# The channel mix's first product by a seven-product scheme, on 768 tokens at a time

## The chip, the cores and the metric

The kernel runs on one core of one Trainium2 chip. The metric is the device time of one execution in microseconds: 827.92 us is the median of three runs of the kernel before (827.59 to 828.11). The profile is of one further execution on the chip.

## The reference

```python
# attention with pooled queries: q, k, v are (4, 8, 1152, 64)
q_pool = q.reshape(B, H, S // 2, 2, D).mean(axis=3)             # 576 queries a head
scores = scale * np.matmul(q_pool, k.transpose(0, 1, 3, 2))
attn = softmax(scores)                                          # max, exp, sum + 1e-9
x = (attn @ v) as (4, 576, 512)                                 # heads side by side
# channel mix on 2304 tokens of 512
mu, var = mean and variance over the 512
xn = (x - mu) / np.sqrt(var + 1e-06) * g_ln
ch = np.maximum(xn @ w_ch1, 0.0) @ w_ch2                        # 512 -> 2048 -> 512
return x + ch
```

All is float32. Each fp32 product of the score and mix stages is made of three products of high and low parts: an operand a is split into a rounded copy a_hi and the rest a_lo = a - a_hi, and a x b becomes hi x hi + hi x lo + lo x hi.

## The kernel before, in words

Attention runs over 16 pairs of heads. The order of TensorE's and ScalarE's steps in a pair is written out in a string (`PAIR_STEPS`, L75): a letter is a step, the number behind @ the PSUM bank, of which there are eight. S is a block of scores, M a block for the row maxima, L and E the rest of the maxima, SH the turn of the maxima, Z the row sums, PV the values, O the turn of the outputs, KA and KQ the keys' and queries' banks (filled by VectorE's transposes), T the turn of a tile of tokens for the mix. Before a step reuses a bank it waits for whoever read the bank last (`pair_free`, L324). VectorE has a list of its own (`VECTOR_STEPS`, L85): m takes maxima, o scales outputs into `x`, a adds two of the exponential tiles, t makes the low parts of turned tokens. GpSimd adds the exponentials up for the row sums (L447). In pairs 2 to 5 it also splits four slices of the mix's weights (L432, L435), and the rest is split by ScalarE and VectorE in the first chunk.

The mix takes 18 tiles of 128 tokens in six chunks of three (384 tokens). For every one of 16 blocks of 128 hidden columns, TensorE makes `up` (L1051: 12 matmuls of 384 columns, into banks 4 or 5), ScalarE the high part of the Relu (L1101), VectorE its low part (L1122), and TensorE, one block later, `down` (L1064: 9 matmuls of 512 columns, summed over all blocks in banks 0, 1 and 7). All the weights stay in SBUF, split. While a chunk runs, its successor's tokens are normalised (L243), turned by TensorE (L251), scaled by g and rounded by ScalarE (`tokens_hi`, L258), and their low parts made by VectorE (`tokens_lo`, L266). The three turns stand behind blocks 6, 9 and 12 and alternate between banks 6 and 2:

```python
TURN_AT = {6: 0, 9: 1, 12: 2}
```

At a chunk's end VectorE adds the three banks to `x` (L1142), and the sync engine stores the tiles. Every engine works through its instructions in the order in which they are written; between engines there are only semaphores.

## Time and profile before

| | |
|---|---|
| median of the runs | 827.92 us (827.59 to 828.11) |
| profiled execution: span, time | 825.7 us, 827.5 us |
| TensorE busy | 812.1 us (98%), 6620 matmuls |
| VectorE busy | 460.5 us (56%) |
| ScalarE busy | 332.7 us (40%) |
| GpSimd busy | 359.0 us (43%) |
| the mix's first matmul starts | 416.0 us |

The span is the time between the first and the last instruction on the chip, the time of the execution holds a little more on both sides. Busy is the time in which an engine has an instruction under way. For matmuls the mean duration of one is its latency; since they overlap, the pitch (busy time over their number, or the chain's pieces) says what one costs.

### The profile page before, as it was taken

To read this page: it belongs to the slowest core of one execution; us is meant where nothing else is said; L and a number is where in the kernel's file an instruction comes from. 1 tells how busy PE (TensorE), PEld (TensorE's weight loads), DVE (VectorE), ACT (ScalarE), POOL (GpSimd) and SP (SyncE) were. 2 spreads that over 40 slices of the span, in tenths; PEclk is the share of its full clock that TensorE was granted. 3 is DMA by queue.
4 is the path that set the end of the run, shared out by engine and by line. 5 is a ranking of instruction groups with operands and counts; after the bars stand their busy time and mean duration, and the time that the engine had idled before them with its cause. 6 is when DMAs were issued, how large, how long until landed. Compare 5 with 4: busy or idle time off the path is not lost.

```text
span 825.7 us, 16074 instructions
## 1 busy us (share of the span) xinstructions
PE 812.1 (98%) x6620; PEld 686.0 (83%) x6620; DVE 460.5 (56%) x705; ACT 332.7 (40%) x717; POOL 359.0 (43%) x252
## 2 busy tenths in 40 slices
PE   8999999999999999999999999999999999999998
PEld 6777777777777877777789999999999999999997
DVE  7888889889989888977254542232223213122112
ACT  4576556576556667555534321211211121111110
POOL 3988999998889888889720000000000000000000
PEclk9999999999999999999999999999999999999999
DMA  8586534456544456310224310010001001001001
GB/s 196 118 194 143 134 96 93 108 143 143 134 100 97 105 138 142 87 31 2 82 77 128 103 39 0 1 39 1 1 1 39 1 0 39 1 1 39 1 1 39
DMA packets 30840, 58.51 MB, mean 71 GB/s; under 512 B 8240, under 2 KB 18736, under 8 KB 27184
## 3 DMA queue, kind: packets, MB, share of 16 engines
q1 hardware_dynamic: 29296, 57.10, 27.5%
q8 instruction: 53, 0.87, 0.5%
q10 hardware_dynamic: 1472, 0.39, 0.2%
q14 instruction: 19, 0.16, 0.1%
HBM read 52.76 MB, written 4.72 MB: 70 GB/s over the span
## 4 chain that ended last, share of the span: by engine, by line
PE 89%; DVE 7%; ACT 2%; issue 2%; DMA 1%; SPq 0%; POOL 0%; DVEq 0%; ACTq 0%; POOLq 0%
PE banks L1051 24%; PE banks L1064 23%; PE banks L594 16%; PE banks L583 10%; PE banks L527 4%; PE banks L581 3%; DVE pm L878 3%; DVE acc_end L902 2%; PE banks L610 2%; ACT pT L781 1%; PE banks L535 1%; PE banks L621 1%; PE banks L251 1%; PE banks L657 1%; DMA k_in_rows<-in_k_dram 1%
## 5 line engine op out<-in xcount | busy, mean ns | idle before, releaser
L447 POOL TENSOR_TENSOR acc<-acc,pT 128x576 f32<-128x576 f32 x160 | 237.5, 1484 | 23.0
L1051 PE MATMUL banks<-xT,weights 128*128 128x384 f32 x1152 | 216.7, 338 | 0.3 <-DVE weights L1113 0.3
L1064 PE MATMUL banks<-weights,hT 128*128 128x512 f32 x864 | 210.7, 389 | 0.0
L1051 PEld LDWEIGHTS banks<-xT,weights 128*128 128x128 f32 x1152 | 201.5, 188 | 7.0 <-DVE weights L1113 0.8
L1122 DVE SCALAR_TENSOR_TENSOR hT<-banks,hT 128x384 fp32r<-128x384 f32 x96 | 53.5, 558 | 274.4 <-ACT hT L1101 274.4
L781 ACT ACTIVATE pT<-banks 128x576 f32<-128x576 f32 x288 | 171.7, 653 | 37.5 <-PE banks L581 31.5
L1064 PEld LDWEIGHTS banks<-weights,hT 128*128 128x128 f32 x864 | 160.9, 188 | 26.9
L1101 ACT ACTIVATE hT<-banks 128x384 fp32r<-128x384 f32 x96 | 47.2, 492 | 323.5 <-PE banks L1051 323.5
L878 DVE TENSOR_REDUCE pm<-banks 128x2 f32<-128x1024 f32 x128 | 153.2, 1221 | 40.0 <-PE banks L527 39.0
L583 PE MATMUL banks<-qT,kT 64*128 64x288 f32 x1728 | 162.1, 298 | 4.7 <-DVE pm L878 3.5
L583 PEld LDWEIGHTS banks<-qT,kT 64*128 64x128 f32 x1728 | 133.4, 184 | 19.9 <-DVE pm L878 8.8
L594 PE MATMUL banks<-pT,vn 128*64 128x288 f32 x1152 | 145.9, 407 | 0.0
L237 POOL TENSOR_TENSOR rstd<-var_eps,minus_half 128x3 f32<-128x3 f32 x6 | 5.5, 916 | 281.6 <-DVE var_eps L232 281.6
L594 PEld LDWEIGHTS banks<-pT,vn 128*64 128x64 f32 x1152 | 80.3, 137 | 56.3 <-issue 5.6
L581 PE MATMUL banks<-shT,ones 64*128 64x288 f32 x576 | 84.7, 290 | 0.0
L527 PE MATMUL banks<-kT,qT 64*128 64x512 f32 (+1 forms) x384 | 62.6, 365 | 1.5 <-DVE pm L878 1.3
L787 ACT COPY oT<-banks 128x288 f32<-128x288 f32 x32 | 12.8, 399 | 106.9 <-PE banks L594 106.9
L447 POOL TENSOR_TENSOR acc<-pT 128x576 f32<-128x576 f32 x32 | 45.4, 1419 | 23.0 <-ACT pT L781 23.0
L581 PEld LDWEIGHTS banks<-shT,ones 64*128 64x128 f32 x576 | 54.2, 184 | 0.0
L451 POOL TENSOR_TENSOR acc<-acc,acc_end 128x576 f32<-128x576 f32 x32 | 50.7, 1583 | 2.5
L902 DVE TENSOR_TENSOR acc_end<-pT 128x576 f32<-128x576 f32 x32 | 42.0, 1313 | 8.9 <-ACT pT L781 8.6
L527 PEld LDWEIGHTS banks<-kT,qT 64*128 64x128 f32 x384 | 32.5, 184 | 10.5 <-issue 7.1
(89 smaller groups left out, 515.3 us busy)
## 6 DMA issues: line engine op xcount, KB each, us to landing
q_in_rows<-in_q_dram SPq DMA_DIRECT2D x56, 284.0 KB, 6.7
k_in_rows<-in_k_dram SPq DMA_DIRECT2D x56, 284.0 KB, 5.2
vn<-in_v_dram SPq DMA_DIRECT2D x16, 576.0 KB, 5.2
wstage<-in_moe_w_ch_dram SPq DMA_DIRECT2D x32, 256.0 KB, 2.9
out_dram<-x SPq DMA_DIRECT2D x16, 256.0 KB, 2.2
q_in_rows<-in_q_dram SPq DMA_DIRECT2D x4, 256.0 KB, 3.1
k_in_rows<-in_k_dram SPq DMA_DIRECT2D x2, 288.0 KB, 4.1
out_dram<-x SPq DMA_DIRECT2D x4, 128.0 KB, 2.4
```

Source lines behind the costliest of these rows:

```text
L447: nc.gpsimd.tensor_tensor(total, pT[:, h % 2, 0] if kt == 1 else total, pT[:, h % 2, kt], ALU.add).then_inc(chained, 1)
L451: nc.gpsimd.tensor_tensor(total, total, acc_end[:], ALU.add).then_inc(acc_ready, 1)
L527: last = nc.tensor.matmul(dst[:, s, col:col + width], qT[rows, j % 2, 0, t * 128:(t + 1) * 128], kT[rows, j % 2, 0, key:key + width], star ...
L581: last = nc.tensor.matmul(dst, ones[rows], shT[rows, queries], start=False, stop=True)
L583: nc.tensor.matmul(dst, kT[rows, j % 2, a, keys], qT[rows, j % 2, b, queries], start=(a, b) == (0, 0), stop=False)
L594: last = nc.tensor.matmul(dst[s * DH:(s + 1) * DH, 0:HW], vn[:, s, kt], pT[:, h % 2, kt, s], start=kt == 0, stop=kt == KT - 1)
L781: nc.scalar.activation(pT[:, h % 2, kt], pair_banks("S", n)[:, :, 0:HW], ACT.Exp, scale=SCALE).then_inc(exp_done, 1)
L878: nc.vector.tensor_reduce(pm[:, at // GROUPS, :, at % GROUPS], src, AX.X, ALU.max).then_inc(max_taken, 1)
L902: nc.vector.tensor_tensor(acc_end[:], pT[:, h % 2, KT - 2], pT[:, h % 2, KT - 1], ALU.add).then_inc(end_added, 1)
L1051: last = nc.tensor.matmul(ps_h[f % 2][:, 0:CW], weights[:, 2 * f, a, c * 128:(c + 1) * 128], xT[:, par, b, c], start=m == 0, stop=m == len ...
L1064: last = nc.tensor.matmul(ps_y[kk], hT[:, f % 2, a, kk * 128:(kk + 1) * 128], weights[:, 2 * f + 1, b], start=f == 0 and m == 0, stop=f == ...
L1122: nc.vector.scalar_tensor_tensor(out=hT[:, f % 2, 1], in0=ps_h[f % 2][:, 0:CW], scalar=0.0, in1=hT[:, f % 2, 0].bitcast(f32), op0=ALU.max, ...
```

## The change

The mix now takes six tiles at a time (a part, 768 tokens, three parts), as two halves of 384 tokens: `xg_a` and `xg_b`. Two blocks of 128 hidden columns form a unit, eight units a part, 24 in all. With A the transposed weights of a unit, cut into 2 x 2 blocks (128 hidden columns by 256 inputs), and B the tokens, cut into 2 x 2 blocks (256 inputs by 384 tokens), the four blocks of A B come from seven block products (`product`, six matmuls each) of the weight forms A11, S2, A12, S1, S3, S4, A22 with the token forms B11, T2, B21, T1, T3, B22, T4. S and T are sums and differences. GpSimd makes the S's of every unit (`sum_weights`), ScalarE rounds each form (`weights_hi`), VectorE makes the rest (`weights_lo`). The seven products use banks 6 and 7 in turn. VectorE adds them up in SBUF (`mid`, by `middle`): "V", "11", "V5", "V7", "22", "12", "21", of which "11", "12", "21", "22" are the four blocks of hidden values. The Relu's high part comes from ScalarE (`hidden_hi`), the low part from VectorE (`hidden_lo`), and `down` makes its four parts of nine matmuls (k = 0 to 3, banks 0 to 2 for even k, 3 to 5 for odd), one unit later.

The weights don't stay in SBUF: each unit's w_up slice (512 KB) and its two w_down slices (256 KB each) are loaded, and split, again in every part. The token forms of a part (`xf`, 7 forms) are made once, in the unit before and the unit behind the border between parts. The tiles of the first part are turned in attention's pairs 12, 13 and 14, those of the others in units 4, 5 and 6 of the part before, two in each, both into bank 7.

Attention itself: the two turns in a pair move to banks 1 and 0 ahead of SH, Z and PV, GpSimd no longer splits weights, the statistics move to pairs 9 and 10 (three tiles each) and the normalisations to pairs 11 to 13 (two each), and VectorE's last pair has a list of its own.

TensorE at the end of attention's pairs 12 and 13. Before (L594 the values, L560 the turn of the maxima, L610 row sums):

```order
L594 MATMUL banks<-pT,vn 64x288 x17
L560 MATMUL banks<-ident,mx 64x128 [waits max_ready,end_taken]
L560 MATMUL banks<-ident,mx 64x128
L610 MATMUL banks<-acc,tile_ones 64x128 [waits acc_ready,rest_taken]
...
L610 MATMUL banks<-acc,tile_ones 64x96 x2
L594 MATMUL banks<-pT,vn 64x288 [waits v_in,exp_done,rest_taken]
```

Now (L687, L653 and L703 are the same three, L266 is the turn of a tile of tokens):

```order
L687 MATMUL banks<-pT,vn 64x288 x17
L266 MATMUL banks<-ident,xn 128x128 [waits xn_ready,rest_taken]
L266 MATMUL banks<-ident,xn 128x128 x3
...
L653 MATMUL banks<-ident,mx 64x128 [waits max_ready,end_taken]
...
L703 MATMUL banks<-acc,tile_ones 64x128 [waits acc_ready,xg_ready]
...
L703 MATMUL banks<-acc,tile_ones 64x96 x2
L687 MATMUL banks<-pT,vn 64x288 [waits v_in,exp_done,xg_ready]
```

Two turns of four transposes stand in between, and row sums and values wait for `xg_ready`, ScalarE's scaling of the turned tiles.

TensorE in the mix, where it turns tokens. Before (L1051 up, L1064 down, L251 the turn):

```order
L1064 MATMUL banks<-weights,hT 128x512 x8
L251 MATMUL banks<-ident,xn 128x128 [waits xt_ready,xn_ready,x_written]
L251 MATMUL banks<-ident,xn 128x128 x3
L1051 MATMUL banks<-xT,weights 128x384 [waits h_ready,w_ready]
L1051 MATMUL banks<-xT,weights 128x384 x11
```

Now, the end of a unit (L1203 a block product, L1213 down, L266 the turn):

```order
L1203 MATMUL banks<-xf,w1f 128x384 [waits mid_made,w1_lo]
L1203 MATMUL banks<-xf,w1f 128x384 x5
L266 MATMUL banks<-ident,xn 128x128 [waits xn_ready,mid_made]
L266 MATMUL banks<-ident,xn 128x128 x3
L1213 MATMUL banks<-w2f,hT 128x512 [waits h_lo,w2_lo]
L1213 MATMUL banks<-w2f,hT 128x512 x8
L266 MATMUL banks<-ident,xn 128x128 [waits xn_ready,xg_ready]
```

There are two turns in a unit, nine matmuls apart, and the second waits for `xg_ready`. What ScalarE does before it signals that (L1286 `hidden_hi`, L368 `weights_hi`, L1296 the second weights, L282 the scaling):

```order
L1286 ACTIVATE hT<-mid 128x384 [waits down_done,mid_made]
L368 CAST w1f<-w_sums 128x256 [waits product_done,sums_made,w1_in1]
L1286 ACTIVATE hT<-mid 128x384 [waits down_done,mid_made]
L368 CAST w1f<-w_sums 128x256 [waits product_done,sums_made,w1_in1] x2
L368 CAST w1f<-w_stage 128x256 [waits product_done,w1_in1]
L1296 CAST w2f<-w_stage 128x512 [waits down_done,w2_in1]
L282 ACTIVATE xg_b<-banks,g_cols 128x128 [waits x_lo5,x_lo2,tokens_summed,x_lo0,xn_turned]
L282 ACTIVATE xg_b<-banks,g_cols 128x128 x3
```

The second Relu is that of "21", the last sum of a unit; five operations stand between it and the scaling's end.

VectorE behind a border. Before (L266 the low part of turned tokens, L1122 the Relu's low part, L1142 the additions to `x`):

```order
L266 SCALAR_TENSOR_TENSOR xT<-banks,g_cols,xT 128x128 x3
L1122 SCALAR_TENSOR_TENSOR hT<-banks,hT 128x384 [waits h_hi]
L1142 TENSOR_TENSOR x<-banks,x 128x512 [waits down_done] x3
L1122 SCALAR_TENSOR_TENSOR hT<-banks,hT 128x384 [waits h_hi]
L223 BN_STATS stats<-x 128x6
```

Now, the end of the first unit of a part (L1349 `middle`, L373 `weights_lo`, L1354 `hidden_lo`, L1360 the second weights' rest, L240 statistics, L1369 the additions):

```order
L1349 TENSOR_TENSOR mid<-banks,mid 128x384 [waits h_lo,mid_made,product_done]
L373 TENSOR_TENSOR w1f<-w_sums,w1f 128x256 [waits w1_hi]
L1354 SCALAR_TENSOR_TENSOR hT<-mid,hT 128x384 [waits h_hi]
L373 TENSOR_TENSOR w1f<-w_sums,w1f 128x256 [waits w1_hi]
L373 TENSOR_TENSOR w1f<-w_stage,w1f 128x256 [waits w1_hi]
L1360 TENSOR_TENSOR w2f<-w_stage,w2f 128x512 [waits w2_hi]
L240 BN_STATS stats<-x 128x6 [waits x_written]
L240 BN_STATS stats<-x 128x6 x2
L1369 TENSOR_TENSOR x<-banks,x 128x512 [waits down_done]
L1369 TENSOR_TENSOR x<-banks,x 128x512 x2
L1354 SCALAR_TENSOR_TENSOR hT<-mid,hT 128x384 [waits h_hi]
L1369 TENSOR_TENSOR x<-banks,x 128x512 [waits down_done]
```

The additions came right behind the chunk's last Relu; now they stand behind eight more operations, and TensorE's `down` of that unit waits for them (`summed`).

The diff, cut to its core:

```diff
-    CT = 3
-    CHUNKS = ALL_TILES // CT
-    CW = CT * 128
+    CT = 6
+    PARTS = ALL_TILES // CT
+    CW = CT // 2 * 128
+    FP = FC // 2
+    UNITS = PARTS * FP
+    FORMS = 7
+    HC = DC // 2
+    W_RING = 9
...
-                  "S@6 M@4 S@0 O@6 E@3 L@0 PV@2 KQ@4 KA@6 T@4 T@5 SH@3 Z@1 PV@0")
+                  "S@6 M@4 S@0 O@6 E@3 L@0 PV@2 T@1 T@0 KQ@4 KA@6 SH@3 Z@1 PV@0")
...
-    TURNS = {PAIRS - 2: (0, 1), PAIRS - 1: (2,)}
+    TURNS = {PAIRS - 4: (0, 1), PAIRS - 3: (2, 3), PAIRS - 2: (4, 5)}
...
+        def sum_weights(eng, vector, u):
+            vector.wait_ge(w1_in[u % 2], 16 * (u // 2 + 1))
+            wait(vector, w1_lo, FORMS * (u - 2) + S4 + 1)
...
+            eng.tensor_tensor(s1, a21, a22, ALU.add).then_inc(sums_made, 1)
+            eng.tensor_tensor(weight_block(u, S3), a11, a21, ALU.subtract).then_inc(sums_made, 1)
+            vector.wait_ge(sums_made, 4 * u + 1)
+            eng.tensor_tensor(s2, s1, a11, ALU.subtract).then_inc(sums_made, 1)
+            vector.wait_ge(sums_made, 4 * u + 3)
+            eng.tensor_tensor(weight_block(u, S4), a12, s2, ALU.subtract).then_inc(sums_made, 1)
...
+        def last_pair_vector(dve):
+            j = PAIRS - 1
+            for i in (T1, T2):
+                sum_tokens(nc.vector, dve, 0, i)
+            tokens_hi(dve, nc.vector.tensor_copy, 0, T2)
+            tokens_hi(dve, nc.vector.tensor_copy, 0, T1)
+            tokens_lo(nc.vector, dve, 0, T2)
+            tokens_lo(nc.vector, dve, 0, T1)
+            add_end(dve, 2 * j)
+            sum_tokens(nc.vector, dve, 0, T3)
+            sum_tokens(nc.vector, dve, 0, T4)
+            take_end(j + 1)
+            scale_outputs(j - 2)
+            add_end(dve, 2 * j + 1)
+            for i in range(FORMS):
+                weights_lo(0, i)
+                if i == S2:
+                    take_end(j + 2)
+                    scale_outputs(j - 1)
+            for i in (B22, T3, T4):
+                tokens_lo(nc.vector, dve, 0, i)
...
+            def product(u, i):
...
+                elif i == 0:
+                    pe.wait_ge(mid_made, mid_made_by(u - 1, "21"))
...
+                elif i == 2:
+                    pe.wait_ge(first_copied, u + 1)
+                elif i > 2:
+                    pe.wait_ge(mid_made, mid_made_by(u, ("V", "11", "V5", "22")[i - 3]))
+                terms = [(a, b, c) for c in range(HC) for a, b in ((0, 0), (0, 1), (1, 0))]
...
+            for u in range(UNITS):
+                turns = turned_in(u)
+                product(u, 0)
+                if u:
+                    down(u - 1, 0)
+                product(u, 1)
+                product(u, 2)
+                if u:
+                    down(u - 1, 1)
+                product(u, 3)
+                if u == 0:
+                    tensor_step(pe, "Z", PAIRS - 1)
+                product(u, 4)
+                if u:
+                    down(u - 1, 2)
+                product(u, 5)
+                product(u, 6)
+                if turns:
+                    pe.wait_ge(mid_made, mid_made_by(u, "12"))
+                    turn_tokens(*turns[0], banks[:, 7])
+                if u:
+                    down(u - 1, 3)
...
+                if turns:
+                    pe.wait_ge(xg_ready, CT * turns[0][0] + turns[0][1] + 1)
+                    turn_tokens(*turns[1], banks[:, 7])
...
+            for u in range(UNITS):
+                n, p = at_border(u), u % FP
+                following = u // FP + 1
+                middle(u, "V")
+                next_lo(u, 0)
...
+                middle(u, "12")
+                next_lo(u, 3)
+                hidden_lo(u, 1)
+                middle(u, "21")
+                next_lo(u, 4)
+                hidden_lo(u, 2)
+                next_lo(u, 5)
+                next_lo(u, 6)
+                if u == 0:
+                    take_end(PAIRS + 2)
+                    scale_outputs(PAIRS - 1)
+                second_lo(2 * u + 1)
+                if following < PARTS:
+                    if p < 2:
+                        dve.wait_ge(x_written, PAIRS)
+                        for kk in range(CT // 2):
+                            statistics(following, CT // 2 * p + kk)
```

## Rows read from the trace of the kernel before

**Rows 1.** The page: busy time of TensorE, and its granted clock in 40 slices.

```profile
PE 812.1 (98%) x6620; PEld 686.0 (83%) x6620; DVE 460.5 (56%) x705; ACT 332.7 (40%) x717; POOL 359.0 (43%) x252
...
PEclk9999999999999999999999999999999999999999
```

**Rows 2.** Groups: line, engine, operation, shapes, count | busy us, mean ns | idle before.

```profile
L1051 PE MATMUL banks<-xT,weights 128*128 128x384 f32 x1152 | 216.7, 338 | 0.3 <-DVE weights L1113 0.3
L1064 PE MATMUL banks<-weights,hT 128*128 128x512 f32 x864 | 210.7, 389 | 0.0
```

**Rows 3.** Window of the second chunk: stretch, length, busy us by engine, clock, DMA.

```profile
483.40:550.70 67.30, 67.30 (x350) 61.51 (x349) 17.55 (x42) 10.96 (x28) 0.85 (x1) 1.00 0.03 12
```

**Rows 4.** Chain of waits, in the mix: start us, us, what.

```profile
450.42 2.08 PE banks L1051 x12
454.55 2.08 PE banks L1051 x12
...
482.30 4.08 PE banks L1064 x18
...
549.68 4.08 PE banks L1064 x18
```

**Rows 5.** Timeline at the handover: start us, us, engine, line, what.

```profile
407.79 7.93 POOL L447 TENSOR_TENSOR acc<-acc,pT 128x576 f32<-128x576 f32 x5
...
411.04 1.14 ACT L258 ACTIVATE xT<-banks,g_cols 128x128 fp32r<-128x128 f32 x4 [0.24 <-PE banks L251]
...
415.79 1.42 POOL L451 TENSOR_TENSOR acc<-acc,acc_end 128x576 f32<-128x576 f32 x1
416.04 2.35 PE L1051 MATMUL banks<-xT,weights 128*128 128x384 f32 x12
```

**Rows 6.** Timeline at the end of the mix.

```profile
817.68 4.24 PE L1064 MATMUL banks<-weights,hT 128*128 128x512 f32 x18
817.88 0.49 ACT L1101 ACTIVATE hT<-banks 128x384 fp32r<-128x384 f32 x1 [3.63 <-PE banks L1051]
```

**Rows 7.** Groups of VectorE, by shape.

```profile
L1122 DVE SCALAR_TENSOR_TENSOR hT<-banks,hT 128x384 fp32r<-128x384 f32 x96 | 53.5, 558 | 274.4 <-ACT hT L1101 274.4
...
L1113 DVE TENSOR_TENSOR weights<-wstage,weights 128x512 fp32r<-128x512 f32 x28 | 18.0, 685 | 2.9 <-ACT weights L1093 2.9
...
L223 DVE BATCH_NORM_STATS2 stats<-x 128x6 f32<-128x512 f32 x18 | 12.1, 683 | 0.0
```

**Rows 8.** Timeline of VectorE: two weight rests without a wait between.

```profile
428.93 1.27 DVE L1113 TENSOR_TENSOR weights<-wstage,weights 128x512 fp32r<-128x512 f32 x2
```

**Rows 9.** Groups of ScalarE, by shape.

```profile
L1101 ACT ACTIVATE hT<-banks 128x384 fp32r<-128x384 f32 x96 | 47.2, 492 | 323.5 <-PE banks L1051 323.5
...
L1093 ACT CAST weights<-wstage 128x512 fp32r<-128x512 f32 x28 | 16.1, 625 | 0.0
...
L733 ACT CAST kT<-banks 128x128 fp32r<-128x128 f32 x16 | 4.6, 285 | 0.0
```

**Rows 10.** A group of GpSimd.

```profile
L457 POOL TENSOR_TENSOR kT<-pT,kT 128x1152 fp32r<-128x1152 f32 x2 | 5.3, 2628 | 4.1 <-ACT pT L756 4.1
```

**Rows 11.** Line L902, VectorE beside GpSimd: ns min/median/max, first and last start.

```profile
L902 DVE TENSOR_TENSOR acc_end<-pT x32: 757/1376/1881, 31.2 to 406.4; 128x576 f32<-128x576 f32 x32
```

**Rows 12.** Chain of waits at the end of pair 13.

```profile
361.45 0.22 PE banks L560 x4
361.67 1.05 PE banks L610 x24
362.72 4.37 PE banks L594 x36
```

**Rows 13.** Chain of waits: the first values of pairs 1, 2 and 3.

```profile
61.39 4.52 PE banks L594 x36
...
85.89 4.52 PE banks L594 x36
...
110.67 4.52 PE banks L594 x36
```

More of the change, by code:

```diff
@@ L256, in tokens_hi @@
             nc.scalar.wait_ge(xn_turned, CT * n + kk + 1)
-            for c in range(DC):
-                last = nc.scalar.mul(xT[:, par, 0, c, kk * 128:(kk + 1) * 128], bank[:, c * 128:(c + 1) * 128],
-                                     g_cols[:, c:c + 1])
-            last.then_inc(xt_hi, 1)
-        def tokens_lo(n, par, kk, bank):
-            nc.vector.wait_ge(xt_hi, CT * n + kk + 1)
-            for c in range(DC):
-                at = slice(kk * 128, (kk + 1) * 128)
-                last = nc.vector.scalar_tensor_tensor(
-                    out=xT[:, par, 1, c, at], in0=bank[:, c * 128:(c + 1) * 128], scalar=g_cols[:, c:c + 1],
-                    in1=xT[:, par, 0, c, at].bitcast(f32), op0=ALU.mult, op1=ALU.subtract)
-            last.then_inc(xt_ready, 1)
+            for i in (B11, B21, B22):
+                wait(nc.scalar, x_lo[i], n)
@@ new lines, in scale_tokens @@
+            wait(nc.scalar, tokens_summed, 4 * n)
+            if n == 0 and kk >= CT // 2:
+                nc.scalar.wait_ge(kq_turned, PAIRS)
+                nc.scalar.wait_ge(ka_turned, PAIRS)
+            half, at = (xg_a, xg_b)[kk // 3], slice(kk % 3 * 128, (kk % 3 + 1) * 128)
+            for c in range(DC):
+                last = nc.scalar.mul(half[:, c, at], bank[:, c * 128:(c + 1) * 128], g_cols[:, c:c + 1])
+            last.then_inc(xg_ready, 1)
+        B11, T2, B21, T1, T3, B22, T4 = range(FORMS)
@@ new lines, in pooled_attention_channel_mix, with sum_tokens @@
+        A11, S2, A12, S1, S3, S4, A22 = range(FORMS)
+        BLOCK_SUMS = (S1, S3, S2, S4)
+        def sum_tokens(eng, vector, n, i):
+            low, high = slice(0, HC), slice(HC, DC)
+            count = 4 * n + (T1, T2, T3, T4).index(i)
+            vector.wait_ge(xg_ready, CT * (n + 1))
+            if i == T1:
+                wait(vector, x_lo[T3], n)
+                out, a, b = token_sums[:, 0], xg_b[:, low], xg_a[:, low]
+            elif i == T2:
+                wait(vector, x_lo[T4], n)
+                out, a, b = token_sums[:, 1], xg_b[:, high], token_sums[:, 0]
+            elif i == T3:
+                vector.wait_ge(x_lo[T1], n + 1)
+                out, a, b = token_sums[:, 0], xg_b[:, high], xg_b[:, low]
+            else:
+                vector.wait_ge(x_lo[T2], n + 1)
+                out, a, b = token_sums[:, 1], xg_a[:, high], token_sums[:, 1]
+            wait(vector, tokens_summed, count)
+            eng.tensor_tensor(out, a, b, ALU.subtract).then_inc(tokens_summed, 1)
@@ L972, in attention_vector @@
+                if j == PAIRS - 6:
                     moments_of(0)
                     variance_eps(0)
[L974 to L976 removed]
+                if PAIRS - 5 <= j < PAIRS - 2:
+                    for kk in range(2):
+                        normalize(0, 2 * (j - PAIRS + 5) + kk)
                 if j == PAIRS - 2:
[L978 to L982 removed]
@@ L1009, in mix_sync @@
[L1009 to L1020 removed]
+                    dve.wait_ge(scored, KT * 2 * (PAIRS - 1))
@@ new lines, in pooled_attention_channel_mix, with mid_made_by, turned_in, at_border @@
+        PRODUCT_BANK = (6, 7, 6, 7, 6, 7, 6)
+        MADE = ("V", "11", "V5", "V7", "22", "12", "21")
+        BLOCKS = ("11", "12", "21", "22")
+        BLOCK_AT = (2, 3, 4, 1)
+        def mid_made_by(u, what):
+            return len(MADE) * u + MADE.index(what) + 1
+        def turned_in(u):
+            n, p = divmod(u, FP)
+            return [(n + 1, kk) for kk in range(2 * p - 8, 2 * p - 6)] if 4 <= p < 7 and n + 1 < PARTS else []
+        def at_border(u):
+            n, p = divmod(u, FP)
+            return n + 1 if p == FP - 1 and n + 1 < PARTS else None
@@ L1021, in mix_sync, with behind_border, load_second_weights, send @@
+        def behind_border(u):
+            return u // FP if u % FP == 0 and u else None
+        def mix_sync(sp):
+            def load_second_weights(m):
+                wait(sp, w2_lo, m - 1)
+                sp.dma_start(w2_stage[:, m % 2], w2_v[:, m % FC]).then_inc(w2_in[m % 2], 16)
+            def send(tile):
                 c, t = tile // TILES, tile % TILES
@@ new lines, in send @@
+                return 16
+            sp.wait_ge(pv_done, HALVES)
+            for m in range(2):
+                load_second_weights(m)
+            sent = 0
+            for u in range(UNITS):
+                if u + 2 < UNITS:
+                    load_first_weights(sp, u + 2)
+                if u + 1 < UNITS:
+                    for m in (2 * u + 2, 2 * u + 3):
+                        load_second_weights(m)
+                if behind_border(u):
+                    sent += sum(send(CT * (u // FP - 1) + kk) for kk in range(CT))
@@ L1171, in _ @@
                 attention_vector(dve)
+                last_pair_vector(dve)
                 mix_vector(dve)
```

530 lines of the change are left out of this document (321 added, 209 removed).

## The prediction

> **What bounds the kernel now.** I began with the shares and slices of the page: TensorE is busy 98% of the span and its granted clock is 9 tenths or more in every slice [rows 1]. The costliest groups say on what: the channel mix's first product (L1051, 1152 matmuls of 384 columns) and its second (L1064, 864 of 512) hold 216.7 and 210.7 us [rows 2]. The window of one chunk says who else works there: in 67.3 us TensorE is busy for 67.3, VectorE for 17.6, ScalarE for 11.0 [rows 3]. So in the mix TensorE alone sets the time, and the others have room. The chain of waits gives pitches: twelve first-product matmuls take 2.08 us (0.174 each), eighteen second-product ones 4.08 (0.227 each), and a chunk 67.38 [rows 4], of which 16 x (2.085 + 2.04) = 66.0 is products and the rest three turns of four transposes, 0.46 each. The whole mix is 416.04 to 821.92, 405.9 us [rows 5, 6].
>
> **What is removed.** Seven block products of 6 matmuls for eight: 42 matmuls a unit of 256 hidden columns and 384+384 tokens, 24 units, 1008 for 1152. 144 x 0.174 = 25.0 us less on TensorE. The second product keeps its 864. TensorE's own work in the mix becomes 1008 x 0.1737 + 864 x 0.227 + 12 turns x 0.46 + 2.2 (last row sums and turns of outputs) = 378.9 us. Were it never to wait, the change would gain 27 us. So the question is only what it waits for.
>
> **Prices of what is added.** VectorE: 384 wide 0.56 us, 512 wide 0.69 [rows 7]; 256 wide lies between, 0.42. Without a wait between them two of 512 take 1.27, so each costs 0.09 less in a row [rows 8]: 0.47, 0.60, 0.34. ScalarE: 0.49 for 384, 0.62 for 512, 0.28 for 128 [rows 9], so 0.39 for 256, again some 0.09 less in a row; a turned tile scaled in four pieces takes 1.14 [rows 5]. GpSimd: 1.59 for 576 [rows 5], 2.63 for 1152 [rows 10], so about 0.75 for 256 and 1.85 for 768. Most new operands lie in SBUF; L1113 and L1093 read SBUF too, so the prices hold for them.
>
> **One steady unit.** TensorE's order is P0 D0 P1 P2 D1 P3 P4 D2 P5 P6 D3 (P 1.04 us, D 2.04): P5 ends at 12.38, P6 at 13.42, the unit at 15.46. Products have two banks, so every product waits for the sum that empties its bank. In the first half there is room (V at 4.3, "11" at 5.4, V5 at 8.5, "22" by 11.1, wanted at 12.4). The tight chain is the last: P5's end is seen 0.2 later (a product's end to its Relu, [rows 6]), "12" 0.56, ScalarE's Relu and the weight copy behind it 0.8, VectorE's weight rest and hidden rest 0.81, "21" 0.56: done at 15.4, and P0 of the next unit wants bank 6 at 15.46. I charge 0.15 us for each of 13 plain units, 2 us. Bounds: 0, and 0.5 a unit.
>
> **The units that turn tokens** (p = 4 to 6 of the first two parts, six in all). Both turns go to bank 7, and the second waits until ScalarE has scaled the first. ScalarE works in order: behind "21" (15.4) come a Relu (0.40), three weight copies (0.93), the second weights' copy (0.52) and only then the scaling (1.14): 18.4. TensorE, with one turn and D3 behind P6, is there at 15.9 and waits 2.6 us. Six times: 15.6 us. With the copies at their 128-wide price it is 2.2 each, with everything at the full price of one 3.2: 13 to 19. Before, successive turns had different banks and three first products between them. This term alone takes over half of the gain.
>
> **The two borders between parts.** In the last unit of a part VectorE makes four low parts of 768 (0.9 each) between its sums; "22" is then ready only at 12.5 and "21" at 16.1: 0.8 us a border. In the unit behind it VectorE's queue is "21", three weight rests, a hidden rest, the second weights' rest: 18.35; then three statistics (1.8, [rows 7]) and only then the additions that empty banks 0 to 2. The first is done at 20.9. D0 of the next unit, for these banks, wants it at 16.5: 4.4 us at the first border; 2.6 at the second, which has no statistics to take. Together 8.6 (5 to 12).
>
> **The handover from attention.** In the last pair VectorE had almost nothing; now it makes sums, high and low parts of 768-wide operands beside GpSimd, which adds until 417.2 [rows 5]. Beside GpSimd such an instruction of 576 took between 0.76 and 1.88 us, median 1.38 [rows 11]. By the median it reaches the seven weight rests at 412 and, with the last three token forms, V of unit 0 only near 421.7 (before's clock), while P2 ends at 419.5: 2.9 us. In unit 0 no D lies between the products, so they run at VectorE's pace: 1.3 us more. D0 waits for the last scaled outputs, which stand behind the weight rests: 2.8 us. Sum 7.0. Bounds: 3 (no contention) and 11.
>
> **Attention.** Three times two token turns now take banks 1 and 0, ahead of row sums (bank 1) and values (bank 0), which then wait for ScalarE's scaling. Now the row sums start 0.22 behind the maxima's turn and the values 1.05 later [rows 12]. With the turns, ScalarE's oT copy and two scalings (0.36 + 1.14 + 1.07 from 361.5, the end of the values) end at 364.1, so the values start at 364.3 instead of 362.7: 1.7 us for pairs 12 and 13; in pair 14, which already had two turns on other banks, 0.85; the turn in pair 15 is gone, -0.45. GpSimd's early weight splits go: their pairs took 24.78 us and the one before them 24.50 [rows 13], 4 x 0.28 = 1.1 gained. Moved statistics and normalisations: +0.3. Net +3.0 (0.5 to 5).
>
> **Sum.** 378.9 + 2 + 15.6 + 8.6 + 7.0 = 412.1 against 405.9: +6.2. With attention's 3.0, +9.2. The end (three additions, stores) is the same. On the profiled execution, span 825.7 and time 827.5, that gives 836.7; the median of the runs is 827.9, so 837.1. 0.2% is 1.7 us, about what a measurement of this kernel can tell from no change.
>
> **A rule beside it.** [Rows 11] show one VectorE form between 0.76 and 1.88 us while GpSimd works. The Trainium skill, SBUF — State Buffer, section on SBUF's two separate sides, says that a VectorE instruction with two SBUF inputs and a GpSimd one exclude each other for a whole instruction. The spread agrees. By that rule a steady unit, too, can lose one GpSimd instruction: a rival below.
>
> **Rivals.**
> - *The lock falls into the tight chain.* GpSimd makes four weight sums a unit, 3.0 us. They wait for a 512 KB load that is asked for some 3 us into the unit; I place them at 8 to 11, where VectorE has a microsecond to spare. If they start at 12 to 14, the two rests in the tight chain wait for one sum: 0.75 in each of 23 units, +14 net of the slack: 851. For it: [rows 11]. Against: the place. 12%.
> - *The clock falls.* It is at its upper level throughout [rows 1], and TensorE hardly waited in the mix [rows 3], so nothing here shows what a wait of 4 us does. If one border and the handover each brought a unit at 1.2 GHz, a unit's work costs 15.5 more: up to 31, at half of that 852. The Trainium skill, TensorE: Matmul & The Clock Gate, part on the HAM clock gate, says that an idle spell throttles TensorE to half; the two long waits are where that would bite. 8%.
> - *Faster.* Instructions between SBUF and SBUF are shorter than I price them. At half the price "21" is ready at 14.3, the turn costs 0.6 instead of 2.6 (-12), the borders 3.5 less, the handover 4 less: 817.6. It becomes faster than before from about half of that effect, instructions a quarter shorter. Against: L1113 and L1093 read SBUF and follow the PSUM line. 6%.
> - *Half of it covered.* The handover and attention's 10 us hide behind GpSimd's or ScalarE's present idle time: 827, no change. For it: VectorE idles most of the last pair. Against: order of the queues. 6%.
> - Forecast, 829.6 to 846: 68%.
>
> Slower is the forecast, the lock and the clock, and the edge of the half-covered case: 89%. Faster 7% (its rival and 1% of the half-covered), same 4%. The range 829 to 852 takes in the lock and leaves out the faster case, the half-covered one and half of the clock's, 16% in all.
>
> **What would show it.** TensorE's matmuls in the mix 1008 and 864; its turns in the mix waiting on ScalarE's scaling six times, 2 to 3 us each; second-product matmuls waiting on VectorE's output additions by 4.4 and 2.6 us behind units 8 and 16; plain units of 15.5 to 15.7 us; a first product that waits on `mid` at the start; attention's values later by 1.7 in two pairs. If the plain units take over 16 us, the tight chain is longer than I read; if the turn waits are under 1 us, my ScalarE prices are wrong, and with them the sign.

## The result: 866.3 us for 828.0, slower by 4.6%

The changed kernel took 866.3 us (863.9 to 867.9), the kernel before 828.0 (827.6 to 828.5): ratio 1.046, interval 1.043 to 1.049. I had forecast 837.1 in a range of 829 to 852. The direction was right, the size was not: of the 38 us I had 9.

The page of after (span 863.8 us, its own time 865.5), the lines that answer to [rows 1, 2]:

```profile
PE 811.1 (94%) x6476; PEld 672.0 (78%) x6476; DVE 660.2 (76%) x1011; ACT 418.9 (49%) x948; POOL 454.8 (53%) x347
...
PE   8999999999999999999689988887998888899998
...
PEclk9999999999999999999889999999999999999999
...
L1213 PE MATMUL banks<-w2f,hT 128*128 128x512 f32 x864 | 220.7, 402 | 8.9 <-DVE x L1369 6.3
L1203 PE MATMUL banks<-xf,w1f 128*128 128x384 f32 x1008 | 201.2, 347 | 15.8 <-DVE mid L1349 15.6
```

The products are as few as the change says, 1008. But TensorE is busy 94% where it was 98, its row has 8s and a 6 in the mix's half, and the 864 second-product matmuls, which the change does not touch, hold 220.7 us instead of 210.7 [rows 2]. So there are two losses: waits, and the same work done more slowly. The waits of TensorE (line and tile, the engine and line waited for, total, times, longest):

```profile
PE banks L1203 <- DVE mid L1349: 15.6, 8, 7.1
PE banks L266 <- ACT xg_a L282: 9.4, 4, 2.4
PE banks L1213 <- DVE x L1369: 6.3, 2, 3.9
PE banks L266 <- ACT xg_b L282: 4.7, 2, 2.4
PE banks L1213 <- DVE x L799: 2.6, 1, 2.6
```

That is 38.6 us of waits: the six turns (9.4 + 4.7), the additions (6.3), the last outputs (2.6), the sums of blocks (15.6). All but three of them, short waits for the sum "22" near the borders, stand where I had looked for one. The other loss shows in the table by stretch (length, busy time of each engine, granted clock, DMA):

```profile
426.00:436.00 10.00, 5.58 (x38) 5.06 (x39) 7.90 (x13) 1.92 (x5) 5.26 (x6) 0.66 0.19 58
436.00:444.00 8.00, 4.22 (x24) 3.37 (x22) 5.85 (x14) 3.87 (x10) 0.00 (x0) 1.00 0.09 28
444.00:449.00 5.00, 4.86 (x16) 4.08 (x17) 2.94 (x5) 0.00 (x0) 0.02 (x1) 0.66 0.52 157
...
510.00:529.80 19.80, 16.98 (x89) 15.12 (x90) 11.30 (x24) 8.45 (x25) 3.07 (x4) 1.00 0.18 54
529.80:534.80 5.00, 5.00 (x20) 4.46 (x19) 1.19 (x3) 2.01 (x7) 1.11 (x2) 0.66 0.52 157
534.80:548.00 13.20, 13.03 (x68) 11.53 (x66) 6.84 (x15) 3.33 (x9) 1.76 (x3) 1.00 0.09 21
548.00:554.00 6.00, 3.81 (x13) 3.58 (x14) 2.72 (x6) 4.55 (x14) 1.55 (x1) 0.72 0.40 132
```

The clock is at its upper level (2.4 GHz) except in spells of half clock (1.2 GHz) that begin in or right behind a wait: the wait of 7.1 us at the handover, the 2.6 at 444.1, and the second and the third turn wait (529.5, 550.2), not the first (510.5). Such spells stand at nine places of the mix, some 3.4 us long each and twice that at the handover. In the first behind a turn, P0 and D0 took from 529.99 to 534.72, 4.73 us for work of 3.1.

The mix lasts from 419.88 to 860.62, 440.7 us instead of my 412.1; it starts 3.84 later than before (forecast 3.0).

**Three places in the trace.** A unit that turns tokens, first VectorE, then ScalarE, then TensorE (start, us, instruction, idle before):

```profile
504.58 0.56 DVE L1349 TENSOR_TENSOR mid<-banks,mid 128x384 f32<-128x384 f32 x1 [0.54 <-PE banks L1203]
506.02 0.42 DVE L373 TENSOR_TENSOR w1f<-w_sums,w1f 128x256 fp32r<-128x256 f32 x1 [0.89 <-ACT w1f L368]
506.36 0.55 DVE L1354 SCALAR_TENSOR_TENSOR hT<-mid,hT 128x384 fp32r<-128x384 f32 x1
506.83 0.55 DVE L1349 TENSOR_TENSOR mid<-banks,mid 128x384 f32<-128x384 f32 x1
```
```profile
507.42 0.53 ACT L1286 ACTIVATE hT<-mid 128x384 fp32r<-128x384 f32 x1 [1.43 <-DVE mid L1349]
...
508.75 0.61 ACT L1296 CAST w2f<-w_stage 128x512 fp32r<-128x512 f32 x1
509.27 1.13 ACT L282 ACTIVATE xg_a<-banks,g_cols 128x128 f32<-128x128 f32 x4
```
```profile
510.46 0.66 PE L266 MATMUL banks<-ident,xn 128*128 128x128 f32 x4 [2.36 <-ACT xg_a L282]
```

VectorE idles 0.89 us for ScalarE's weight copy while "21" is next but two; everything behind "21" on ScalarE is late by it and by the two rests. The handover, VectorE beside GpSimd, and TensorE:

```profile
419.63 1.54 DVE L373 TENSOR_TENSOR w1f<-w_stage,w1f 128x256 fp32r<-128x256 f32 x1
421.09 4.07 DVE L373 TENSOR_TENSOR w1f<-w_sums,w1f 128x256 fp32r<-128x256 f32 x3
...
427.34 2.34 DVE L337 TENSOR_TENSOR xf<-token_sums,xf 128x768 fp32r<-128x768 f32 x2
429.71 0.56 DVE L1349 TENSOR_TENSOR mid<-banks,mid 128x384 f32<-128x384 f32 x1
```
```profile
414.46 8.00 POOL L542 TENSOR_TENSOR acc<-acc,pT 128x576 f32<-128x576 f32 x5
422.54 1.48 POOL L546 TENSOR_TENSOR acc<-acc,acc_end 128x576 f32<-128x576 f32 x1
...
426.68 1.32 POOL L360 TENSOR_TENSOR w_sums<-w_stage,w_sums 128x256 f32<-128x256 f32 x1
```
```profile
430.42 2.26 PE L1203 MATMUL banks<-xf,w1f 128*128 128x384 f32 x6 [7.10 <-DVE mid L1349]
...
444.14 3.83 PE L1213 MATMUL banks<-w2f,hT 128*128 128x512 f32 x9 [2.60 <-DVE x L799]
```

A weight rest costs 0.42 where GpSimd is idle (row 506.02), here 1.36 to 1.54. V, the first sum, comes at 429.7, not at the 425.5 that my 421.7 makes with the start 3.84 later. GpSimd's row sums, which ended at 417.2 before (421.0 with the same shift), last until 424.0, and weight sums follow until 428.0. And the border behind unit 7:

```profile
566.91 1.85 POOL L313 TENSOR_TENSOR token_sums<-xg_b 128x768 f32<-128x768 f32 x1 [6.91 <-issue]
568.93 1.81 POOL L313 TENSOR_TENSOR token_sums<-xg_a,token_sums 128x768 f32<-128x768 f32 x1 [0.17 <-POOL token_sums L313]
```
```profile
568.97 2.18 DVE L1354 SCALAR_TENSOR_TENSOR hT<-mid,hT 128x384 fp32r<-128x384 f32 x1
571.07 0.55 DVE L1349 TENSOR_TENSOR mid<-banks,mid 128x384 f32<-128x384 f32 x1
```
```profile
571.77 1.29 PE L1203 MATMUL banks<-xf,w1f 128*128 128x384 f32 x6 [2.33 <-DVE mid L1349]
...
593.81 0.47 PE L1213 MATMUL banks<-w2f,hT 128*128 128x512 f32 x1 [3.94 <-DVE x L1369]
```

A hidden rest, 0.55 elsewhere, takes 2.18 beside GpSimd's token sum, in the tight chain right ahead of "21". I had priced that border's chain with GpSimd idle.

### The profile page after: what moved, and what is told of

Read it like the earlier page. It is cut to its first block and busy times, and to the rows that moved or that the text cites. A ratio compares the mean times of both kernels' runs of the same rounds, so it can differ in the third digit from the quotient of the medians.

```text
span 863.8 us, 17118 instructions
## 1 busy us (share of the span) xinstructions
PE 811.1 (94%) x6476; PEld 672.0 (78%) x6476; DVE 660.2 (76%) x1011; ACT 418.9 (49%) x948; POOL 454.8 (53%) x347
## 5 line engine op out<-in xcount | busy, mean ns | idle before, releaser
L1213 PE MATMUL banks<-w2f,hT 128*128 128x512 f32 x864 | 220.7, 402 | 8.9 <-DVE x L1369 6.3
L1203 PE MATMUL banks<-xf,w1f 128*128 128x384 f32 x1008 | 201.2, 347 | 15.8 <-DVE mid L1349 15.6
L1203 PEld LDWEIGHTS banks<-xf,w1f 128*128 128x128 f32 x1008 | 181.9, 193 | 28.6 <-issue 22.8
L1213 PEld LDWEIGHTS banks<-w2f,hT 128*128 128x128 f32 x864 | 166.4, 195 | 39.6 <-issue 7.1
L1286 ACT ACTIVATE hT<-mid 128x384 fp32r<-128x384 f32 x96 | 50.5, 526 | 270.0 <-DVE mid L1349 270.0
L1349 DVE TENSOR_TENSOR mid<-banks,mid 128x384 f32<-128x384 f32 x168 | 93.2, 555 | 77.3 <-PE banks L1203 73.8
L676 PEld LDWEIGHTS banks<-qT,kT 64*128 64x128 f32 x1728 | 133.5, 185 | 18.8 <-DVE pm L987 7.6
L687 PE MATMUL banks<-pT,vn 128*64 128x288 f32 x1152 | 145.9, 407 | 0.0
L355 POOL TENSOR_TENSOR w_sums<-w_stage 128x256 f32<-128x256 f32 x23 | 18.5, 804 | 207.8 <-DMA w_stage<-in_moe_w_ch_dram 207.8
L687 PEld LDWEIGHTS banks<-pT,vn 128*64 128x64 f32 x1152 | 80.3, 137 | 56.2 <-issue 5.6
L373 DVE TENSOR_TENSOR w1f<-w_sums,w1f 128x256 fp32r<-128x256 f32 x96 | 46.5, 486 | 61.3 <-ACT w1f L368 61.3
L1354 DVE SCALAR_TENSOR_TENSOR hT<-mid,hT 128x384 fp32r<-128x384 f32 x96 | 64.6, 673 | 2.9 <-ACT hT L1286 2.6
```

What stands on the lines that cost most here:

```text
L676: nc.tensor.matmul(dst, kT[rows, j % 2, a, keys], qT[rows, j % 2, b, queries], start=(a, b) == (0, 0), stop=False)
L687: last = nc.tensor.matmul(dst[s * DH:(s + 1) * DH, 0:HW], vn[:, s, kt], pT[:, h % 2, kt, s], start=kt == 0, stop=kt == KT - 1)
L1203: last = nc.tensor.matmul(banks[:, PRODUCT_BANK[i], 0:CW], w1f[:, m % W_RING, a, c], xf[:, i, b, c], start=at == 0, stop=at == len(terms) - 1)
L1213: last = nc.tensor.matmul(banks[:, k % 2 * (CT // 2) + kk], hT[:, k, a, tokens], w2f[:, (2 * u + k // 2) % 4, b], start=p == 0 and k < 2 a ...
L1349: nc.vector.tensor_tensor(mid[:, at], banks[:, PRODUCT_BANK[i], 0:CW], mid[:, other], ALU.add).then_inc(mid_made, 1)
L1354: nc.vector.scalar_tensor_tensor(out=hT[:, k, 1], in0=mid[:, BLOCK_AT[k]], scalar=0.0, in1=hT[:, k, 0].bitcast(f32), op0=ALU.max, op1=ALU. ...
```

## Experiments

All are edits of the changed kernel; times are medians, with the range in brackets; n = 4 for each.

**1. Each suspected wait by itself.** Scaling the first turned tile ahead of the weight copies:

```diff
                 next_hi(u, 3)
+                if turns:
+                    scale_tokens(*turns[0], banks[:, 7])
                 hidden_hi(u, 2)
 ...
                 second_hi(2 * u + 1)
-                if turns:
-                    scale_tokens(*turns[0], banks[:, 7])
```


> ScalarE scales the first turned tile of a unit ahead of the Relu of '21' instead of four copies behind it; all else as in the changed kernel. Theory (the wait is one of order): the six waits of 2.36 us before the second turn vanish, 14.2 us, and with them the stretches at the lower clock that follow two of the three in each part, some 1.5 us each of four: 866.3 becomes 846 to 850. Rival (ScalarE and VectorE have too much to do in these units, the order is not at fault): the wait turns up again before P0 or P2 of the next unit, and the time falls by less than 5 us.

846.2 us (845.7 to 846.8): 20.1 faster. The turn waits, 14.1 us, are gone, and the 1872 matmuls hold 414.1 us instead of 421.9, since fewer of them run at half clock (mean clock 0.99 for 0.98). Of that, 3.8 us came back as waits for block sums (19.4 for 15.6).

The additions to `x` ahead of "12", and the statistics a unit later:

```diff
+                if behind_border(u):
+                    dve.wait_ge(down_done, 4 * u - 1)
+                    for kk in range(CT // 2):
+                        add_outputs(CT * (u // FP - 1) + kk)
                 if n:
                     tokens_lo(nc.vector, dve, n, T1)
                 middle(u, "12")
```


> VectorE adds output tiles 0 to 2 right behind '22' in the unit behind a border, and takes the statistics one unit later (units 1 and 2 of a part instead of 0 and 1). Theory: the waits of 3.94 and 2.36 us before D0 of units 9 and 17 shrink to under 0.5, '21' of that unit comes 0.8 later (the additions lie before '12'), the lower clock behind both goes (1.5 us each): 6 to 9 us less than 866.3. Rival: the additions only move the wait to P0, less than 3 us.

862.3 us (860.9 to 863.9): 4.0 faster. The waits of 3.94 and 2.36 us went, but 1.15 us came at the sum that now stands behind the additions, and 0.3 to 0.6 where the statistics went: all waits together fell by 1.1 us only. The larger part of the gain lies in the matmuls, 418.5 us for 421.9.

GpSimd's token sums for the next part held back until "21":

```diff
                 if n:
+                    pool.wait_ge(mid_made, mid_made_by(u, "21"))
                     sum_tokens(nc.gpsimd, pool, n, T3)
```


> At the two borders GpSimd waits for '21' before it makes the token sums T3 and T4. Theory (GpSimd's instruction blocks the hidden rest L1354, which took 2.18 us there instead of 0.55): the hidden rest in the tight chain is back at 0.55, the wait before P0 of units 8 and 16 falls from 2.33 and 2.37 us to about 0.8, so 3 us less, and 1.5 more at the second border where the lower clock followed: 861 to 864. Rival (VectorE's own four low parts of 768 make the wait): no change at these places.

867.2 us (865.2 to 867.4): no gain. TensorE and VectorE of this run:

```profile
571.36 1.29 PE L1204 MATMUL banks<-xf,w1f 128*128 128x384 f32 x6 [0.23 <-DVE mid L1350]
...
581.45 2.35 PE L1204 MATMUL banks<-xf,w1f 128*128 128x384 f32 x12 [2.58 <-DVE mid L1350]
```
```profile
575.50 2.07 DVE L373 TENSOR_TENSOR w1f<-w_sums,w1f 128x256 fp32r<-128x256 f32 x1
577.49 2.05 DVE L373 TENSOR_TENSOR w1f<-w_stage,w1f 128x256 fp32r<-128x256 f32 x1
```

The wait of 2.33 fell to 0.23, so GpSimd's sum was its cause. But GpSimd's work now lies beside the next unit's rests (2.07 for 0.42) and the wait came back there as 2.58. The expectation took the wait for gone where it only moved.

Issuing V's operands first, the last three token rests behind it:

```diff
-            for i in (B22, T3, T4):
-                tokens_lo(nc.vector, dve, 0, i)
 ...
                 middle(u, "11")
+                if u == 0:
+                    tokens_lo(nc.vector, dve, 0, T3)
```


> In unit 0 VectorE makes the low parts of T3, B22 and T4 between the sums instead of ahead of V. Theory (order of VectorE's queue): V comes at 426 instead of 429.7, the wait before P3 falls from 7.1 to about 3.4; the low parts then lie between the sums, 2 us of it come back before P4 to P6: 1 to 3 us less than 866.3, 1.5 of which from the clock. Rival (the handover is bound by the amount of work, not its order): no change within 1 us.

861.4 us (861.0 to 864.8): 4.9 faster, more than either theory; the 7.10 fell to 3.42.

**2. The clock by itself.** Dummy transposes of the identity into a free bank fill the waits (20 at each turn, 60 at the handover, 18 to 32 at the borders); no operation of the kernel changes.

```diff
+                    pe.wait_ge(mid_made, mid_made_by(u, "21"))
+                    filler(20, 6)
                     pe.wait_ge(xg_ready, CT * turns[0][0] + turns[0][1] + 1)
```


> TensorE fills its long waits with transposes whose result nobody reads: 20 before each second turn, 60 before P3 of unit 0, 18 before P0 of units 8 and 16, 32 and 18 before D0 of units 8 and 16. No wait is made shorter. Theory (part of the loss is the clock, which was at its lower level for some 3.4 us behind eight of the waits): the granted clock stays at 1.00, and every product runs at 0.174: 10 to 13 us less than 866.3, the waits themselves as long as before. Rival (the granted clock falls for another reason than idle time, or the work behind a wait was slow for lack of data): the time stays within 3 us or rises by the fillers that overrun the waits.

855.5 us (855.0 to 856.3), mean clock 0.997: 10.8 faster with every wait still there: the six turning units take 19.05 to 19.07 us each, where after has 19.05 to 19.12 for four of them and 20.64 and 20.86 for the two in which a spell lies. This is what the half-clock spells cost, net: one spell is left (at 443.4), and at the borders some of the dummy work runs longer than the wait that it fills.

**3. The contention by itself.** GpSimd's additions for the last pair run over 8 of 288 columns, so its row sums are left out but for these.

> GpSimd's additions for the row sums of the last pair run over 8 of 288 columns (the row sums of that pair are left out but for those), all else as in the changed kernel. Theory (GpSimd's instructions block VectorE's in the last pair and push V of unit 0 from 422 to 429.7): VectorE's instructions there fall to their times alone, 0.95 us for 768 and 0.42 for 256, the wait before P3 of unit 0 falls from 7.1 us to under 1, the lower clock there goes: 8 to 11 us less than 866.3. Rival (ScalarE's copies or the loads are late, or VectorE simply has too much to do): the wait stays above 4 us.

857.2 us (856.6 to 859.2): 9.1 faster. VectorE's line that answers to the row at 421.09:

```profile
418.19 1.09 DVE L373 TENSOR_TENSOR w1f<-w_sums,w1f 128x256 fp32r<-128x256 f32 x3
```

Three rests take 1.09 us instead of 4.07, V starts at 422.4 instead of 429.7, and the wait of 7.10 is gone.

**4. What a product is worth.** P0 issued twice, so eight products:

> The first product of every unit is issued twice (the same result is written again), so that TensorE has eight products a unit again: 144 matmuls more. Theory (outside its waits the mix is TensorE's, and a product not made is worth its full time): 24 x 1.05 = 25 us more, less some 1 us each in the two waits for the output additions: 888 to 892. Rival (the units run at VectorE's or ScalarE's pace, the seven-product scheme saves little): 5 to 12 us more.

877.9 us (876.5 to 881.3): 11.6 slower, not 25. Plain units grew by the full 1.07 us (15.71 to 16.78), but a longer TensorE stretch swallows waits (the additions' 6.3 us fell to 4.3, the block sums' 15.6 to 13.4, the outputs' 2.6 to 1.5) and the mean clock rose from 0.98 to 0.992.

**5. Together.** Edits e1, e2 and e6:

> The early scaling, the early additions with later statistics, and V first in unit 0, together. Theory: the three act on different waits, so they add: 20.1 + 4.0 + 2 less than 866.3, about 840. Rival (they share VectorE's and ScalarE's time): under 20 less.

838.8 us (838.6 to 840.3), 27.5 less than the changed kernel, where the three gave 20.1, 4.0 and 4.9 alone. Then unit 0's weight rests 4 to 6 behind V, and the last outputs scaled right behind "21":

> This is the kernel with the three reorderings (838.8 us) with one more, in unit 0 alone: the first-product weight rests 4 to 6 are taken after V instead of ahead of it, and the last pair's outputs are scaled right behind middle 21 instead of behind weight rests 4 to 6 of the next unit. Theory (what is left of the handover's loss is VectorE's queue, since TensorE waited 3.41 us before P3(0), then 1.69, 0.96 and 2.58 us): V comes three rests of about 1.5 us each earlier only if GpSimd does not stretch what is left, so P3's wait falls to 1 to 2 and the 2.58 to about 1.2; 834 to 837. Rival (GpSimd's sum, not VectorE's order, sets the time of the last of these waits): at most 1 us less, 837.5 to 839.

834.9 us (834.7 to 835.5), 3.9 less. The borders rearranged instead (turns in units 3 to 5, GpSimd's six token rests given to VectorE, its first two token sums earlier and the other two behind "21"):

> The kernel with the three reorderings (838.8 us) with the borders (units 7 to 9 and 15 to 17) rearranged: the tokens are turned in units 3 to 5 of a part instead of 4 to 6, the statistics all stand in unit 1, GpSimd takes the sums T1 and T2 in unit 6 ahead of its weight sums and T3, T4 behind middle 21 of unit 6, and VectorE instead of GpSimd takes the rests of B22, T3 and T4, spread over units 7 and 8. Theory (the borders' waits, 6.6 us at each, are the next part's preparation crowded into the tail of one unit, on two engines that stretch each other): they fall to 1 to 2 us at each border, 829 to 832. Rival (the work only moves, as it did when GpSimd's sums alone were put later): within 2 us of 838.8.

837.6 us (836.0 to 839.3), 1.2 less, where I expected 7 to 10: the rival. Waits moved from the sum "21" to V5 and "22" (1.72 and 1.36 us), which now stood behind token rests on VectorE. All waits for block sums fell by 3.4 us (20.9 to 17.5), but the clock did not gain (mean 0.992 for 0.994). Both:

> Both of these on top of the three reorderings. If the losses of handover and borders are separate queues, the two gains add: 826 to 829, so level with the kernel before (828.0), which would put the scheme's whole deficit of 38 us on order. Rival (a rest of the deficit is work, not order: 2.5 us of pitch in plain units, 3.8 in attention, the handover's own sums): 830 to 835.

835.3 us (833.7 to 835.8), not 826 to 829. In all of these I had moved rests about, and each time a sum stood behind one. So the next kernel put the sums first (diff against e11, units past 0):

```diff
                     hidden_lo(u, 0)
+                    middle(u, "V5")
                     if n:
                         tokens_lo(nc.vector, dve, n, T2)
-                middle(u, "V5")
 ...
                 middle(u, "22")
+                if n:
+                    tokens_lo(nc.vector, dve, n, B21)
                 middle(u, "12")
+                middle(u, "21")
+                if behind_border(u): ...  # the additions to x
                 next_lo(u, 3)
                 hidden_lo(u, 1)
-                middle(u, "21")
```


> The kernel with handover and borders reordered (835.3 us), with VectorE's sums of blocks put ahead of its rests. In every unit 21 stands right behind 12, ahead of the first-product weight rest 3 and the hidden rest 1 (VectorE waited there 0.89 us on ScalarE with the next sum behind it). In the crowded units V5, V7 and 22 stand ahead of B21's rest, the second weight's rest and the additions to x, and in unit 0 V5, V7 and 22 ahead of all that belongs to unit 1. No operation is added or removed. Theory (all of what is left is sums queued behind rests that nobody needs yet): TensorE's waits of 3.40, 1.75 and 0.85 us in unit 0 go to 1.5 together, the borders' 5.3 us each to 1 to 2, and the half clock behind them goes: 820 to 825, faster than the kernel before (828). Rival (a rest of the deficit is engine time, not order: the rests moved behind the sums are then late themselves, as in the two late-sums and border kernels): 832 to 837.

**818.2 us** (817.9 to 819.2), ratio to the kernel before 0.988 (0.987 to 0.990): 1.2% faster than the kernel before, with an interval clear of 1, and faster than the changed kernel, and below my forecast for it. Its page and its waits:

```profile
PE 795.2 (97%) x6476; PEld 662.6 (81%) x6476; DVE 662.3 (81%) x1017; ACT 418.8 (51%) x948; POOL 445.8 (55%) x341
...
PEclk9999999999999999999999999999999999999999
...
L1220 PE MATMUL banks<-w2f,hT 128*128 128x512 f32 x864 | 213.1, 392 | 0.1
L1210 PE MATMUL banks<-xf,w1f 128*128 128x384 f32 x1008 | 195.1, 339 | 8.0 <-DVE mid L1356 6.7
```
```profile
PE banks L1210 <- DVE mid L1356: 6.7, 10, 1.4
PE banks L1210 <- DVE w1f L385: 1.1, 1, 1.1
```

Waits of 38.6 us became 7.8, and the same 1872 matmuls take 408.2 us instead of 421.9. The work is that of the changed kernel, but six token rests are now VectorE's instead of GpSimd's (x1017 and x341 for x1011 and x347), as in the two border orders above.

**6. The last questions.** P0 twice again, in this order:

> The kernel with the sums ahead (818.2 us) with the first of the seven block products issued twice (the second start overwrites the first, nothing else changes), so eight products of columns in the new order. It measures what a product is worth on TensorE where little waits: in the changed kernel the same edit cost 11.6 us, since waits took up the rest. Theory (order was the whole loss): 24 units by 1.07 us, less the 6.7 us of waits that a longer TensorE stretch can swallow: 19 to 25 us, so 837 to 843. Rival (another engine is by now close to being the bound, VectorE at 76% of the span): 8 to 15 us, 826 to 833.

836.9 us (836.5 to 837.2): 18.7 slower, at the edge of the first theory (837) and clearly not the rival's 826 to 833. The starts of P0 in two plain units, of e12 and of e13:

```profile
758.41 1.21 PE L1210 MATMUL banks<-xf,w1f 128*128 128x384 f32 x6
...
774.00 1.21 PE L1210 MATMUL banks<-xf,w1f 128*128 128x384 f32 x6
```
```profile
756.71 1.21 PE L1211 MATMUL banks<-xf,w1f 128*128 128x384 f32 x6
...
773.35 1.21 PE L1211 MATMUL banks<-xf,w1f 128*128 128x384 f32 x6
```

15.59 and 16.64: 1.05 us a unit, 25.2 in all, less what the waits took up (7.8 us in e12, 2.5 here). The rest, 1.2, I did not trace.

And in the changed kernel one line alone, "21" right behind "12":

```diff
                 middle(u, "12")
+                middle(u, "21")
                 next_lo(u, 3)
                 hidden_lo(u, 1)
-                middle(u, "21")
```


> The changed kernel (866.3 us) with one line moved in the units: the sum 21 right behind 12, ahead of the first-product weight rest 3 and the hidden rest 1. Nothing else of the reorderings. In the changed kernel 12 starts at 504.58 us and 21 at 506.83, with VectorE waiting on ScalarE between; product 6 is done about 505.7. Theory (the chain 12, 21, Relu, copies, scaled tokens sets the turn waits): each turn wait of 2.36 us loses about 1.1 us, 6.7 us over the six units, and with waits of 1.3 us the clock holds there, 3 to 6 us more: 853 to 860. Rival (product 6 ends too late, so 21 can't start earlier): 864 to 867.

842.6 us (842.4 to 845.7): **23.7 faster**, well past both ranges. VectorE, TensorE and the stretch of the second turn in this run:

```profile
503.50 0.56 DVE L1349 TENSOR_TENSOR mid<-banks,mid 128x384 f32<-128x384 f32 x1 [0.50 <-PE banks L1203]
```
```profile
507.14 0.66 PE L266 MATMUL banks<-ident,xn 128*128 128x128 f32 x4 [1.18 <-ACT xg_a L282]
```
```profile
523.00:541.00 18.00, 16.83 (x88) 14.99 (x87) 10.68 (x23) 7.85 (x24) 3.06 (x4) 1.00 0.19 59
```

The first row is "21": it starts 13.73 us into its unit (P0 at 489.77) where after has 15.01 (506.83, P0 at 491.82). The turn waits halved (14.1 to 7.0 us in all). By units, the two profiled executions differ by 19.8 us: 10.8 in the six turning units, 6.0 at the borders (the wait of 2.33 for "21" is gone there, and 1.6 of it is back in the unit behind), 1.8 at the handover and 1.2 in the ten plain units (15.71 to 15.59). Of these, 10.0 are in the same matmuls: 214.9 and 197.0 us, where after has 220.7 and 201.2. With turn waits of 1.2 us in the same places the clock stayed up. I had allowed 3 to 6 us for it, and nothing for borders and plain units. The other 4 us lie between executions: the profiled one was e14's slowest (845.7 us, mean clock 0.990), the other three took 842.4 to 842.7 at 0.996.

## Why the prediction was wrong

The mix took 28.6 us more than forecast. By the prediction's own terms, each from the pitches of the units in the traces of after and of e4, in which dummy work keeps the clock up; the first row is not measured but taken over, and the others are what is left above it:

| term | forecast | measured | with the clock held (e4) |
|---|---|---|---|
| products, turns, last rows | 378.9 | 378.9 | 378.9 |
| plain units | 2.0 (0.15 each) | 2.5 (0.25 each) | 2.5 |
| six turning units | 15.6 | 19.5, of it waits 14.1 | 16.1 |
| borders (units 7 to 9, 15 to 17) | 8.6 | 24.3, of it waits 13.5 | 18.8 |
| handover | 7.0 | 15.6, of it waits 11.0 | 14.3 |
| attention | +3.0 | +3.8 | |

Three steps failed. The sum held the clock at its upper level throughout; it took the sum "21" at the borders to be made beside an idle GpSimd (waits of 2.33 and 2.37 us for 0.8); and it put the first wait at the handover at 2.9 us where it was 7.10. In the trace of after TensorE works 30.7 us at half clock, which loses 15.3; waits are 7.4 longer than forecast (4.9 at the borders, 4.0 at the handover, 1.5 less at the turns); the pitch of 15.71 for 15.46 makes 3.7. That is 26.4 of the 28.6; 2.2 are unplaced. The net cost of the clock is less than 15.3: with it held, some waits that the slow work had hidden are back, so e4 gained 10.8.

- **Work removed:** right. 1008 products, 1.05 us for a block product in a plain unit (e12 against e13).
- **Engine prices and the plain unit:** right. 0.42, 0.55 and 0.69 on VectorE, 0.40, 0.61 and 1.13 on ScalarE, for the 0.42, 0.56, 0.69, 0.39, 0.62 and 1.14 that [rows 7 to 9] gave. Only the Relu was longer, 0.53 for 0.49.
- **Turn waits:** right in mechanism and size, 2.36 us each for 2.6 (my own terms add up to 2.5). e1 took them away.
- **The clock.** The sum held every second at the upper level and gave the clock a rival at 8%, tied to the two longest waits. It falls behind waits of 2.4 us too, though not behind each, and it ran through turning units, borders and handover: 10.8 us by e4, 10.0 in the matmuls of e14. That [rows 1] have no low slice says nothing on this, since TensorE hardly waited there.
- **The handover:** three waits named, two right (1.32 for 1.3, 2.60 for 2.8). The one for V was mis-sized. The price of a rest was not the fault: the median of [rows 11], 1.38 for 576 columns, fits the 1.36 to 1.54 measured, although the rests have 256 columns, less than half. The time beside GpSimd was. VectorE came to the seven rests when I had said (415.4, for 412 with the start 3.84 later), but seven rests and three token forms at 1.38 are 13.8 us, and my 412 to 421.7 leaves 9.7; it comes out only if nothing is stretched any more once GpSimd's row sums end at 417.2. They ended 3.0 us later than that in the shifted time, with weight sums right behind them, and VectorE took 14.3 us up to V. Without GpSimd's additions V comes 7.3 us earlier, and the kernel gains 9.1 (e5).
- **Borders:** I named two waits at each (0.8, and 4.4 or 2.6). The additions came about as said, 3.94 and 2.36. The 0.8, for "21" at the next P0, was 2.33 and 2.37: I had priced that chain with GpSimd idle, although the diff puts its token sums there (e3 took the wait to 0.23 and brought it back a few products later). And "22" came late for P6 three times (0.75 and 1.00 in units 7 and 8, 0.76 in unit 15), of which I had 0.1 in units 7 and 15 and left it out: I followed the queue to the first late sum and not on from there.
- **The lock in plain units** did not occur: GpSimd's weight sums fall 7 to 11 us into the unit, where I had placed them, and the pitch stays 15.71.
- **Attention:** right, 3.84 for 3.0; at the end of pair 13 the second run of value matmuls starts 7.57 us behind the first (358.53, 366.10), before 5.68 (356.87, 362.55): 1.9 late, for my 1.7.

The deeper miss is in what I asked of the order. I took it as given and found the chain "12", rest, rest, "21" tight; I did not ask what stood in it that nobody waits for. One line of order was worth 23.7 us, and the scheme, 38 us slower as written, is 9.6 us faster than the kernel before once the sums go first (e12, with the other reorderings).

## What to carry to other kernels

Where TensorE has to wait for another engine to empty its banks, the instructions that empty them go ahead of all others in that engine's queue, above all ahead of ones that wait for a third engine. Price a recurring wait with the clock that may fall behind it: here a third to a half of what e1 and e14 gained was clock. And a saving on an engine that already waits is first eaten by its waits: an eighth product cost 11.6 us in the bad order and 18.7 in the good one.
